# Weaving a gated-scan attention into an MLP's matmuls: k copied ahead of the angle rounding, attention's TensorE work in three groups per slot, x split ahead of the mixing, a second buffer for normalised x

## The chip, the cores and the metric

The kernel runs on one core of one Trainium2 chip. The metric is the device time of one execution in microseconds (us). PE is TensorE, ACT is ScalarE, DVE is VectorE, POOL is GpSimd and SP is the engine whose queue issues the loads and stores. Every engine works through its own instructions in the order of the program; engines wait for each other by semaphores alone.

## The reference

Three layers in a row, all in float32: an attention with a complex gate whose state is carried over time, a mixer with a token MLP and a channel MLP, and a second channel MLP behind a layer norm.

```
# attention: batch 4, heads 8, time 768, head 48
mag = sqrt(a_re**2 + a_im**2); scale = minimum(mag, 0.999) / (mag + 1e-6)
for t: S = (a_t * S) + k_t v_t^T (complex a_t, per row of S);  y_t = q_t @ S.real
x = y as [4, 768, 384]
# mixer
u = x + (relu(x^T @ w_tok1) @ w_tok2)^T          # 768 -> 256 -> 768
x2 = u + relu(u @ w_ch1) @ w_ch2                 # 384 -> 1536 -> 384
# second MLP
xn = (x2 - mean) / sqrt(var + 1e-6) * g_ln
out = x2 + relu(xn @ w2_ch1) @ w2_ch2
```

## The kernel before

**Tiles.** Time is cut into tiles of 128 steps, six (`NT`) to a batch of four, so there are 24 tiles n. For a tile, ACT and DVE compute the gate's running product (a logarithm, a scan, exponentials) and its running angle (an arctangent, a scan, a rounding, two sines), and with them "hats", q and k turned and scaled. SP lays the hats out anew (`rows<-hats`, six transfers a tile). PE then does for each half (`part`) of the eight heads: `turn_k` (k transposed into PSUM bank 6, which ACT copies to `khat`: `keep_khat`) and `scores` (q times k into PSUM bank 5, which DVE masks: `mask`); then `outputs` for each half, and `chunk_state` (DVE's `add_state` reads it). There is one bank for each, so `turn_k(n, 1)` waits for `keep_khat(n, 0)` and `scores(n, 1)` for `mask(n, 0)`. `keep_x` copies the result into the tile of x.

**Passes.** Matmuls of the MLPs have both operands split into a rounded part and a rest, and go in three passes (lines 330, 331, 332 of `split_passes`). ACT rounds (`round_x`, `relu_hidden`, `round_piece` for weights), DVE makes the rest (`rest_x`, `rest_hidden`, `rest_piece`).

**Order.** It is written out by hand for each engine. First the attention of batch 0. Then for each batch b: `mix_tokens(b)` (the token MLP and the transposes of u), and the 24 steps m of the channel MLP, `up(m)` and `down(m)`. The first three MLPs carry the attention of the next batch: one tile n = 6(b+1)+j is a **slot** j of four steps. In it PE interleaves four ups and four downs with the tile's parts; ACT and DVE call `slot`, where `step(i)` is `relu_hidden` or `rest_hidden` of step i, and `prepare(n + 1, ...)` and `prepare(n + 2, ...)` are parts of the gate for the next two tiles. Slots are n = 6 to 23: n = 6 to 11 in batch 0, 12 to 17 in batch 1, 18 to 23 in batch 2. ACT needs one set of tables for logarithm and exponential (`use_logs`) and one for arctangent and sine (`use_turns`), and loads each once a slot.

At a slot's end ACT has `log_magnitude`, `growth` and `angle` for tile n + 2, and DVE `log_sums` between them. The next slot begins on ACT with `relu_hidden(m)`, and on DVE with `rest_hidden(m)`, `turn_scan` (which waits for the arctangent) and only then `mask(n, 0)`. In the fourth slot of a batch (j = 3) DVE also does `add_u` and `row_stats`.

**Mixing.** `mix_down` needs the split of each tile of x; for batches 1 to 3 the split is made at the start of `mix_tokens`, into the space that u's split held.

**Second MLP.** For each batch, `normalise(kk, g)` writes three tiles of normalised x into `xn`, which PE transposes (`turn_xn`). The second half g = 1 uses the same `xn`, so it waits until PE has transposed the first.

Of the kernel before, what the change touches and what calls it, by code (L numbers as in the profile page):

```python
# [13 lines left out]
P = 128  # L14


def gated_scan_mixer_mlp_kernel(nc, q, k, v, a_re, a_im, w_tok1, w_tok2, w_ch1, w_ch2, g_ln, w2_ch1, w2_ch2,
# [43 lines left out]
    with ctx:  # L61
# [52 lines left out]
        raw_ch2b = alloc(m_ctx, "raw_ch2b", [P, FT * C])  # L114
        m_ctx.close()
# [65 lines left out]
        xn = by_tile(plain_tok[:, :, :].rearrange("p n c -> p (n c)")[:, 2 * COLS:2 * COLS + ST * C])  # L181
# [147 lines left out]
        def split_passes(ps, lhs_h, lhs_l, rhs_h, rhs_l, first, final):  # L329
            nc.tensor.matmul(ps, lhs_h, rhs_h, start=first, stop=False, skip_group_check=True)  # L330
            nc.tensor.matmul(ps, lhs_h, rhs_l, start=False, stop=False, skip_group_check=True)  # L331
            return nc.tensor.matmul(ps, lhs_l, rhs_h, start=False, stop=final, skip_group_check=True)  # L332

# [253 lines left out]
        def _(act):  # L587
# [107 lines left out]
            def slot(n, step, slow):  # L695
                step(0)
                prepare(n + 1, round_turns)
                keep_khat(n, 0)
                step(1)
                prepare(n + 1, sines)  # L700
                keep_khat(n, 1)
                prepare(n + 1, decays)
                step(2)
                use_logs()
                prepare(n + 2, square, inverse_of_re)
                step(3)
                prepare(n + 2, log_magnitude)
                keep_x(n, slow)
                prepare(n + 2, growth)
                use_turns()  # L710
                prepare(n + 2, angle)

            def mix_tokens(b):
                if b:
                    for j in range(NT):
                        round_x(b * NT + j)
                for rt in range(RT):
                    act.wait_ge(tok1_done, b * RT + rt + 1)
                    nc.scalar.activation(r1_h[:, rt, :], r1_ps(b)[rt][:, 0:C], ACT.Relu).then_inc(tok_hidden_rounded, 1)
                if b == 0:  # L720
                    use_logs()
                    square(5)
                    round_piece(act, 2)
                    inverse_of_re(5)
                    log_magnitude(5)
                    round_piece(act, 5)
# [4 lines left out]
                if b == 0:  # L731
                    growth(5)
                    use_turns()
                    angle(5)
# [126 lines left out]
        def _(dve):  # L861
# [95 lines left out]
            def rest_x(n):  # L957
                b, j = divmod(n, NT)
                dve.wait_ge(x_rounded, n + 1)
                nc.vector.tensor_tensor(xs_l[:, j, :], x_tile(b, j), xs_h[:, j, :].bitcast(F32), ALU.subtract).then_inc(x_split, 1)  # L960
# [6 lines left out]
            def slot(n, step):  # L967
                step(0)
# [56 lines left out]
            def normalise(kk, g):  # L1025
                b = ORDER[kk]
                dve.wait_ge(rstd_ready, 1 if kk != 1 else 2)
                if kk == 1:
                    dve.wait_ge(x2_kept, B * NT)
                else:  # L1030
                    dve.wait_ge(x2_loaded[kk % 2], 16 * NT * (1 + kk // 2) if kk % 2 == 0 else 16 * NT)
                if kk or g:
                    dve.wait_ge(xn_turned, kk * 2 * CT + g * CT)
                for st in range(ST):
                    j = g * ST + st
                    nc.vector.tensor_scalar(xn[:, st, :], x_tile(kk, j), mean_var[:, b, 2 * j:2 * j + 1], rstd_all[:, b, j:j + 1],
                                            ALU.subtract, ALU.mult).then_inc(xn_ready, 1)
# [9 lines left out]
            def mix_tokens(b):  # L1047
                if b:
                    for j in range(NT):
                        rest_x(b * NT + j)  # L1050
                    add_u(2 * b - 1)
# [17 lines left out]
                if b:  # L1069
                    row_stats(2 * b - 1)  # L1070
                else:
                    rest_piece(dve, 5)
                    log_sums(5)
# [91 lines left out]
            for m in range((B - 1) * STEPS, LAST):  # L1165
# [10 lines left out]
                if kk < 0:  # L1176
# [4 lines left out]
                    if s == 8:  # L1181
                        rstd(0, slice(0, B - 1))
                        normalise(0, 0)
                    if 12 <= s < 18:
                        rest_turned(0, s - 12)
                        if s == 14:
                            normalise(0, 1)
                    if s == STEPS - 1:
                        rest_piece(dve, 2 + PER_MLP + CT)
                else:  # L1190
# [6 lines left out]
                    if kk + 1 < B:  # L1197
                        if s == 5:
                            normalise(kk + 1, 0)
                        if 7 <= s < 13:  # L1200
                            rest_turned(kk + 1, s - 7)
                            if s == 9:
                                normalise(kk + 1, 1)
# [3 lines left out]
        def _(pe):  # L1207
# [98 lines left out]
            def turn_xn(kk, i):  # L1306
# [6 lines left out]
                for st in range(ST):  # L1313
                    last = nc.tensor.transpose(turn2_ps[ct][:, st * P:(st + 1) * P], xn[:, st, ct * P:(ct + 1) * P], ident[:, :])  # L1314
                last.then_inc(xn_turned, 1)

            def mix_down(b, rt, j):
                pe.wait_ge(x_split, b * NT + j + 1)
                last = split_passes(r1_ps(b)[rt][:, 0:C], tok1_h[:, j, rt * P:(rt + 1) * P], tok1_l[:, j, rt * P:(rt + 1) * P],
                                    xs_h[:, j, :], xs_l[:, j, :], j == 0, j == NT - 1)  # L1320
                if j == NT - 1:
                    last.then_inc(tok1_done, 1)

            def mix_tokens(b):
# [3 lines left out]
                for rt in range(RT):  # L1328
                    for j in range(NT) if b else (NT - 1,):
# [40 lines left out]
            for b in range(B):  # L1370
                mix_tokens(b)
                first = b * STEPS
                if b + 1 < B:
                    for j in range(NT):
# [17 lines left out]
                        down(m + 1)  # L1392
                        chunk_state(n)
# [67 lines left out]
```

## Time and profile before

| | |
|---|---|
| median of 3 runs | 970.07 us (969.06 to 970.95) |
| profiled execution | 970.12 us, span 968.3 us |
| PE busy | 886.5 us (92%) |
| DVE busy | 469.7 us (49%) |
| ACT busy | 414.9 us (43%) |
| POOL busy | 21.6 us (2%) |
| mean granted TensorE clock | 0.981 |

PE is busy nearly all the time, so what the time depends on is where PE stands still, and on whom it then waits. The attention of batch 0 takes the first 128 us. Weaved slots run from 142 to 555 us with two mixings between them, and after 571 us PE has only MLP steps, with the transposes of normalised x.

### The profile page before, as it was taken

To read this page: it belongs to the slowest core of one execution; us is meant where nothing else is said; L and a number is where in the kernel's file an instruction comes from. 1 tells how busy PE (TensorE), PEld (TensorE's weight loads), DVE (VectorE), ACT (ScalarE), POOL (GpSimd) and SP (SyncE) were. 2 spreads that over 40 slices of the span, in tenths; PEclk is the share of its full clock that TensorE was granted. 3 is DMA by queue.
4 is the path that set the end of the run, shared out by engine and by line. 5 is a ranking of instruction groups with operands and counts; after the bars stand their busy time and mean duration, and the time that the engine had idled before them with its cause. 6 is when DMAs were issued, how large, how long until landed. Compare 5 with 4: busy or idle time off the path is not lost.

```text
span 968.3 us, 13819 instructions
## 1 busy us (share of the span) xinstructions
PE 886.5 (92%) x5600; PEld 868.4 (90%) x5600; DVE 469.7 (49%) x821; ACT 414.9 (43%) x767; POOL 21.6 (2%) x39
## 2 busy tenths in 40 slices
PE   0768887899999999999999999899999999999998
PEld 0657777889999999989999999899999999999998
DVE  5866456656558557566665354425312322322121
ACT  6766356665655656646665332222211211211111
POOL 1000000000000000000000000000000000000000
PEclk9979897999999999999999999999999999999999
DMA  9826953434442544534436070000002002000000
GB/s 370 175 42 99 257 103 44 87 74 97 94 99 37 111 76 98 92 81 75 74 58 113 3 269 1 1 1 1 26 1 74 1 25 74 1 25 25 1 25 25
DMA packets 46834, 70.99 MB, mean 73 GB/s; under 512 B 5040, under 2 KB 38064, under 8 KB 46256
## 3 DMA queue, kind: packets, MB, share of 16 engines
q1 hardware_dynamic: 46768, 70.09, 31.2%
q8 instruction: 44, 0.72, 0.3%
q14 instruction: 22, 0.18, 0.1%
HBM read 42.86 MB, written 8.26 MB: 53 GB/s over the span
## 4 chain that ended last, share of the span: by engine, by line
PE 74%; DVE 11%; ACT 7%; DMA 4%; issue 2%; SPq 2%; DVEq 0%; ACTq 0%
PE bank L330 20%; PE bank L332 20%; PE bank L331 20%; PE bank L1229 3%; PE bank L1248 3%; DMA rows<-hats 3%; PE bank L1246 3%; PE bank L1220 2%; DMA x_u<-in_re_rows_dram 1%; PE bank L1259 1%; SPq L463 1%; ACT L594 1%; PE bank L1212 1%; DVE turned_x L1068 1%; PE bank L1314 1%
## 5 line engine op out<-in xcount | busy, mean ns | idle before, releaser
L984 DVE SCALAR_TENSOR_TENSOR hidden<-bank,hidden 128x384 fp32r<-128x384 f32 x192 | 106.9, 557 | 347.9 <-ACT hidden L693 347.8
L693 ACT ACTIVATE hidden<-bank 128x384 fp32r<-128x384 f32 x192 | 93.8, 488 | 347.8 <-PE bank L332 347.3
L330 PE MATMUL bank<-ch,hidden 128*128 128x384 f32 x576 | 198.5, 345 | 0.0
L332 PE MATMUL bank<-ch,hidden 128*128 128x384 f32 x576 | 194.1, 337 | 0.0
L331 PE MATMUL bank<-ch,hidden 128*128 128x384 f32 x576 | 193.9, 337 | 0.0
L330 PEld LDWEIGHTS bank<-ch,hidden 128*128 128x128 f32 x576 | 109.2, 190 | 0.4 <-issue 0.3
L331 PEld LDWEIGHTS bank<-ch,hidden 128*128 128x128 f32 x576 | 109.2, 190 | 0.0
L332 PEld LDWEIGHTS bank<-ch,hidden 128*128 128x128 f32 x576 | 109.0, 189 | 0.0
L330 PE MATMUL bank<-turned_x,ch 128*128 128x384 f32 x288 | 102.3, 355 | 1.9 <-DVE turned_x L1068 1.9
L332 PE MATMUL bank<-turned_x,ch 128*128 128x384 f32 x288 | 97.3, 338 | 0.0
L331 PE MATMUL bank<-turned_x,ch 128*128 128x384 f32 x288 | 97.2, 337 | 0.0
L1212 PE MATMUL bank<-ident_r 128*128 128x512 f32 x110 | 42.8, 473 | 28.8 <-DVE hats L930 28.8
L1246 PE MATMUL bank<-v_t,scratch 128*128 128x48 f32 x384 | 67.1, 266 | 0.0
L1246 PEld LDWEIGHTS bank<-v_t,scratch 128*128 128x128 f32 x384 | 62.3, 195 | 1.1
L1248 PE MATMUL bank<-state,rows 96*128 96x48 f32 x320 | 62.3, 277 | 0.0
L1220 PE MATMUL bank<-ident,rows 96*128 96x96 f32 x192 | 26.7, 264 | 33.7 <-ACT scratch L660 29.6
L330 PEld LDWEIGHTS bank<-turned_x,ch 128*128 128x128 f32 x288 | 54.7, 190 | 2.8 <-issue 2.3
L1220 PEld LDWEIGHTS bank<-ident,rows 96*128 96x128 f32 x192 | 20.3, 147 | 40.5 <-ACT scratch L660 32.2
L331 PEld LDWEIGHTS bank<-turned_x,ch 128*128 128x128 f32 x288 | 54.7, 190 | 0.0
L332 PEld LDWEIGHTS bank<-turned_x,ch 128*128 128x128 f32 x288 | 54.5, 189 | 0.0
L1229 PE MATMUL bank<-rows 96*128 96x128 f32 x384 | 54.4, 287 | 0.0
L938 DVE TENSOR_TENSOR scratch<-bank,causal 128x512 f32<-128x512 f32 x48 | 33.1, 689 | 43.2 <-PE bank L1229 43.2
(165 smaller groups left out, 1555.0 us busy)
## 6 DMA issues: line engine op xcount, KB each, us to landing
rows<-hats SPq DMA_DIRECT2D x126, 128.5 KB, 4.6
a_t<-in_a_rows_dram SPq DMA_DIRECT2D x20, 384.0 KB, 4.0
qk_t<-in_qk_rows_dram SPq DMA_DIRECT2D x19, 384.0 KB, 5.6
v_t<-in_v_cols_dram SPq DMA_DIRECT2D x24, 192.0 KB, 4.1
plain_ch<-in_moe_w_ch_dram SPq DMA_DIRECT2D x6, 768.0 KB, 10.8
out_dram<-x_u SPq DMA_DIRECT2D x24, 192.0 KB, 2.0
x_kept_dram<-x_u SPq DMA_DIRECT2D x18, 192.0 KB, 3.2
x_u<-x_kept_dram SPq DMA_DIRECT2D x18, 192.0 KB, 3.2
```

The costliest lines, as they stand in the source:

```text
L330: nc.tensor.matmul(ps, lhs_h, rhs_h, start=first, stop=False, skip_group_check=True)
L331: nc.tensor.matmul(ps, lhs_h, rhs_l, start=False, stop=False, skip_group_check=True)
L332: return nc.tensor.matmul(ps, lhs_l, rhs_h, start=False, stop=final, skip_group_check=True)
L463: sp.dma_start(rows[r * D + g * DD:r * D + (g + 1) * DD, n % 2, :, :], hats_of(n)[:, r, g, :]).then_inc(rows_landed[n % 2], 16)
L693: nc.scalar.activation(hid_h[:, m % NHID, :], hid_ps[m % 2][:, 0:HALF], ACT.Relu).then_inc(hidden_rounded, 1)
L938: nc.vector.tensor_tensor(masked[:, part * 512:(part + 1) * 512].rearrange("p (h t) -> p h t", h=HB), scored[:, :].rearrange("p (h t) -> p ...
L984: nc.vector.scalar_tensor_tensor(out=hid_l[:, m % NHID, :], in0=hid_ps[m % 2][:, 0:HALF], scalar=0.0, in1=hid_h[:, m % NHID, :].bitcast(F3 ...
L1212: nc.tensor.matmul(banks[0][:, :], ident_r[:, :], ident_r[:, :].unsqueeze(1).to_broadcast([P, 4, P]), start=True, stop=True)
L1220: last = nc.tensor.transpose(turned[:, g * D2:(g + 1) * D2], rows[:, n % 2, part * HB + g, P:2 * P], ident[0:D2, 0:D2])
L1229: last = nc.tensor.matmul(scored[:, g * P:(g + 1) * P], rows[:, n % 2, part * HB + g, P:2 * P], rows[:, n % 2, part * HB + g, 0:P], start= ...
L1246: last = nc.tensor.matmul(yh, masked[:, h * P:(h + 1) * P], v_head(n, h), start=True, stop=n % NT == 0)
L1248: last = nc.tensor.matmul(yh, rows[:, n % 2, h, 0:P], state[:, n % 2, h * D:(h + 1) * D], start=False, stop=True)
```

## The change

PE gets another order in a slot. Before, `turn_k` and `scores` of each half, the two `outputs` and `chunk_state` stood apart between ups and downs; now they stand in three groups: `turn_k` and `scores` of half 0; the same of half 1; and both `outputs` with `chunk_state`. The third `up` and `down` stand ahead of that last group, and the slot's fourth `up` behind it.

ACT copies `khat` ahead of `round_turns`, and keeps x ahead of step 3. In slot n = 6 the piece of weights 5 and the growth and angle of tile 7 move out of `mix_tokens(0)` to behind the first copy of k. DVE adds the state ahead of step 3. The split of x goes from the start of the mixing into the slots j = 3 and j = 5 (even tiles first, then, behind step 3, the odd ones), and `mix_down` goes through tiles in that order, both halves (`rt`) of each in turn. `xn` becomes two buffers, one for each half, and both halves are normalised in neighbouring steps (8 and 9, then 4 and 5).

```diff
+        xn_second = alloc(m_ctx, "xn_second", [P, ST * C])
...
+        def mix_order(b):
+            return (*range(0, NT, 2), *range(1, NT, 2)) if b else range(NT)
...
@@ ACT
             def slot(n, step, slow):
+                b, j = divmod(n, NT)
                 step(0)
-                prepare(n + 1, round_turns)
                 keep_khat(n, 0)
-                step(1)
-                prepare(n + 1, sines)
-                keep_khat(n, 1)
-                prepare(n + 1, decays)
+                if j == ST:
+                    for i in range(0, ST, 2):
+                        round_x(b * NT + i)
+                if j == NT - 1:
+                    round_x(b * NT + j - 1)
+                if n == NT:
+                    round_piece(act, 5)
+                    growth(n + 1 - PAIRS)
+                    use_turns()
+                    angle(n + 1 - PAIRS)
+                    step(1)
+                    keep_khat(n, 1)
+                    prepare(n + 1, round_turns)
+                else:
+                    prepare(n + 1, round_turns)
+                    step(1)
+                    keep_khat(n, 1)
+                prepare(n + 1, sines, decays)
                 step(2)
                 use_logs()
                 prepare(n + 2, square, inverse_of_re)
+                keep_x(n, slow)
                 step(3)
-                prepare(n + 2, log_magnitude)
-                keep_x(n, slow)
-                prepare(n + 2, growth)
+                if j == NT - 1:
+                    for i in range(1, NT, 2):
+                        round_x(b * NT + i)
+                prepare(n + 2, log_magnitude, growth)
                 use_turns()
                 prepare(n + 2, angle)
...
@@ DVE
             def slot(n, step):
+                b, j = divmod(n, NT)
                 step(0)
-                prepare(n + 1, turn_scan)
-                mask(n, 0)
-                step(1)
-                prepare(n + 1, turns_wrapped)
-                mask(n, 1)
+                if n == NT:
+                    mask(n, 0)
+                    rest_piece(dve, 5)
+                    mask(n, 1)
+                    prepare(n + 1, turn_scan)
+                    step(1)
+                    prepare(n + 1, turns_wrapped)
+                else:
+                    prepare(n + 1, turn_scan)
+                    mask(n, 0)
+                    if j == ST:
+                        for i in range(0, ST, 2):
+                            rest_x(b * NT + i)
+                    if j == NT - 1:
+                        rest_x(b * NT + j - 1)
+                    step(1)
+                    prepare(n + 1, turns_wrapped)
+                    mask(n, 1)
                 prepare(n + 1, grown_qk)
                 step(2)
                 prepare(n + 1, turn_hats)
                 prepare(n + 2, abs2)
+                add_state(n)
                 step(3)
+                if j == NT - 1:
+                    for i in range(1, NT, 2):
+                        rest_x(b * NT + i)
                 prepare(n + 2, ratio0, ratio_step, log_sums)
-                add_state(n)
...
@@ PE
-                for rt in range(RT):
-                    for j in range(NT) if b else (NT - 1,):
+                for j in mix_order(b) if b else (NT - 1,):
+                    for rt in range(RT):
                         mix_down(b, rt, j)
...
                         turn_k(n, 0)
+                        scores(n, 0)
                         up(m + 1)
-                        scores(n, 0)
                         turn_k(n, 1)
+                        scores(n, 1)
                         if j:
                             down(m - 1)
-                        scores(n, 1)
                         up(m + 2)
+                        down(m)
                         outputs(n, 0)
-                        down(m)
+                        outputs(n, 1)
+                        chunk_state(n)
                         up(m + 3)
-                        outputs(n, 1)
                         down(m + 1)
-                        chunk_state(n)
```

On PE, in a slot in the middle of batch 1's MLP, these rows stood before (L1220 is `turn_k`, L1229 `scores`, L1246 `outputs`, L1259 `chunk_state`; an `up` reads `turned_x`, a `down` reads `hidden`; of each group the first row):

```order
L1220 MATMUL bank<-ident,rows 128x96 [waits khat_kept,rows_landed0]
...
L330 MATMUL bank<-turned_x,ch 128x384 [waits hidden_split]
...
L1229 MATMUL bank<-rows 128x128 [waits state_sums]
...
L1220 MATMUL bank<-ident,rows 128x96 [waits khat_kept]
...
L1229 MATMUL bank<-rows 128x128 [waits scores_masked]
...
L1246 MATMUL bank<-v_t,scratch 128x48 [waits states_decayed,scores_masked,x_kept,loaded_v0]
...
L1259 MATMUL bank<-v_t,scratch 96x48 [waits khat_kept,scores_masked]
```

And these stand there now (L1248 is `turn_k`, L1257 `scores`, L1274 `outputs`, L1287 `chunk_state`):

```order
L1248 MATMUL bank<-ident,rows 128x96 [waits khat_kept,rows_landed0]
...
L1257 MATMUL bank<-rows 128x128 [waits state_sums]
...
L331 MATMUL bank<-turned_x,ch 128x384 [waits hidden_split]
...
L1248 MATMUL bank<-ident,rows 128x96 [waits khat_kept]
...
L1257 MATMUL bank<-rows 128x128 [waits scores_masked]
...
L1274 MATMUL bank<-v_t,scratch 128x48 [waits states_decayed,scores_masked,x_kept,loaded_v0]
...
L1287 MATMUL bank<-v_t,scratch 96x48 [waits khat_kept,scores_masked]
L331 MATMUL bank<-turned_x,ch 128x384 [waits hidden_split]
```

The first scores moved ahead of an up, the second scores ahead of a down, and the slot's last up from ahead of the second outputs to behind the chunk's state.

On ACT, from the end of one slot into the next, these rows stood before (L624 is `growth`, L632 `angle`, L693 the ReLU, L637 `round_turns`, L660 `keep_khat`):

```order
L672 ACTIVATE x_u<-bank 128x384 [waits outputs_ready]
L624 ACTIVATE grow<-scratch 128x384 [waits grown,log_sums_done]
L625 ACTIVATE grow<-scratch 128x384
L594 ACT_TABLE_LOAD
L632 ACTIVATE scratch<-scratch 128x384 [waits hats_done,ratio_done]
L693 ACTIVATE hidden<-bank 128x384 [waits hidden_used,hidden_ready]
L637 ACTIVATE scratch<-scratch,round_bias 128x384 [waits turn_sums]
L660 ACTIVATE scratch<-bank 128x384 [waits k_turned]
```

And these stand there now (the same operations, at L632, L640, L701, L668 and L645; L680 is `keep_x`):

```order
L680 ACTIVATE x_u<-bank 128x384 [waits outputs_ready]
L701 ACTIVATE hidden<-bank 128x384 [waits hidden_used,hidden_ready]
...
L632 ACTIVATE grow<-scratch 128x384 [waits grown,log_sums_done]
L633 ACTIVATE grow<-scratch 128x384
L602 ACT_TABLE_LOAD
L640 ACTIVATE scratch<-scratch 128x384 [waits hats_done,ratio_done]
L701 ACTIVATE hidden<-bank 128x384 [waits hidden_used,hidden_ready]
L668 ACTIVATE scratch<-bank 128x384 [waits k_turned]
L645 ACTIVATE scratch<-scratch,round_bias 128x384 [waits turn_sums]
```

The copy of k moved ahead of the rounding, and x is kept one step earlier; growth, table load, angle and the next slot's first ReLU stand in the order in which they stood.

## Rows read from the trace of the kernel before

**Rows 1.** Waits of PE over the whole span: total, times, longest in us

```profile
PE bank L1220 <- ACT scratch L660: 29.6, 10, 8.3
...
PE bank L1314 <- DVE plain_tok L1036: 6.6, 4, 2.7
...
PE bank L1220 <- DMA rows<-hats: 4.0, 5, 1.5
PE bank L330 <- DVE turned_x L960: 3.9, 3, 1.8
...
PE bank L330 <- DVE hidden L1054: 0.6, 1, 0.6
```

**Rows 2.** Timeline of PE around slot n = 14: start, duration, tile, shapes, count

```profile
333.55 0.42 PE L330 MATMUL bank<-turned_x,ch 128*128 128x384 f32 x1
...
349.07 0.32 PE L1246 MATMUL bank<-v_t,scratch 128*128 128x48 f32 x2
...
353.73 0.42 PE L330 MATMUL bank<-turned_x,ch 128*128 128x384 f32 x1
...
356.94 0.49 PE L1220 MATMUL bank<-ident,rows 96*128 96x96 f32 x4
...
361.85 1.06 PE L1229 MATMUL bank<-rows 96*128 96x128 f32 x8
```

**Rows 3.** Timeline of ACT over the same slot's end

```profile
349.27 0.49 ACT L693 ACTIVATE hidden<-bank 128x384 fp32r<-128x384 f32 x1 [1.32 <-PE bank L332]
...
353.56 0.52 ACT L624 ACTIVATE grow<-scratch 128x384 f32<-128x384 f32 x1 [1.24 <-DVE scratch L893]
...
354.52 1.28 ACT L594 ACT_TABLE_LOAD   x1
355.81 0.52 ACT L632 ACTIVATE scratch<-scratch 128x384 f32<-128x384 f32 x1
356.24 0.47 ACT L693 ACTIVATE hidden<-bank 128x384 fp32r<-128x384 f32 x1
...
359.32 0.47 ACT L660 ACTIVATE scratch<-bank 128x384 f32<-128x384 f32 x1
```

**Rows 4.** Timeline of DVE over the same slot's end

```profile
351.97 0.56 DVE L888 SCALAR_TENSOR_TENSOR scratch<-scratch 128x384 f32<-128x384 f32 x1
...
357.81 0.96 DVE L905 TENSOR_TENSOR_SCAN scratch<-keep,scratch 128x384 f32<-128x384 f32 x1
360.05 0.69 DVE L938 TENSOR_TENSOR scratch<-bank,causal 128x512 f32<-128x512 f32 x1 [1.29 <-PE bank L1229]
```

**Rows 5.** Timeline: the tile's hats on DVE, and PE's wait for their rows

```profile
368.46 1.81 DVE L930 TENSOR_TENSOR hats<-qk_t,scratch 128x768 f32<-128x768 f32 x2
...
378.02 0.55 PE L1220 MATMUL bank<-ident,rows 96*128 96x96 f32 x4 [0.74 <-DMA rows<-hats]
```

**Rows 6.** Timeline of PE in batch 0's MLP: first up, two waits, the tenth tile's slot

```profile
142.28 0.44 PE L330 MATMUL bank<-turned_x,ch 128*128 128x384 f32 x1 [0.19 <-DVE turned_x L1068]
...
153.06 0.90 PE L1220 MATMUL bank<-ident,rows 96*128 96x96 f32 x4 [6.10 <-ACT scratch L660]
...
200.24 0.90 PE L1220 MATMUL bank<-ident,rows 96*128 96x96 f32 x4 [2.36 <-ACT scratch L660]
...
215.83 0.42 PE L330 MATMUL bank<-turned_x,ch 128*128 128x384 f32 x1
```

**Rows 7.** Timeline of ACT and DVE there: a piece of weights rounded, and its rest

```profile
153.27 1.48 ACT L322 ACTIVATE ch<-plain_ch 128x1536 fp32r<-128x1536 f32 x1
...
154.79 1.76 DVE L327 TENSOR_TENSOR ch<-plain_ch,ch 128x1536 fp32r<-128x1536 f32 x1 [0.81 <-ACT ch L322]
```

**Rows 8.** Stretches: length, busy of PE, PEld, DVE, ACT, POOL, granted clock, DMA

```profile
202.00:204.00 2.00, 2.00 (x10) 2.00 (x8) 0.00 (x0) 1.78 (x6) 0.00 (x0) 0.59 0.00 0
280.00:282.00 2.00, 1.09 (x6) 1.12 (x7) 1.79 (x4) 2.00 (x6) 0.00 (x0) 1.00 0.00 0
618.00:619.00 1.00, 0.67 (x5) 0.68 (x6) 0.27 (x1) 0.00 (x0) 0.00 (x0) 1.00 0.00 0
```

More of the change, by code:

```diff
@@ L332, in split_passes, with splits_through @@
             return nc.tensor.matmul(ps, lhs_l, rhs_h, start=False, stop=final, skip_group_check=True)
+        def mix_order(b):
+            return (*range(0, NT, 2), *range(1, NT, 2)) if b else range(NT)
+        def splits_through(n):
+            b, j = divmod(n, NT)
+            return b * NT + list(mix_order(b)).index(j) + 1
         def links(n):
@@ L713, in mix_tokens @@
             def mix_tokens(b):
-                if b:
-                    for j in range(NT):
-                        round_x(b * NT + j)
                 for rt in range(RT):
@@ L730, in mix_tokens @@
                     nc.scalar.activation(u_h[:, ct, g * HALF:(g + 1) * HALF], turn_ps[i][:, 0:HALF], ACT.Copy).then_inc(u_rounded, 1)
[L731 to L734, printed above, removed]
             def log_variances(i, bs):
@@ L958, in rest_x @@
                 b, j = divmod(n, NT)
-                dve.wait_ge(x_rounded, n + 1)
+                dve.wait_ge(x_rounded, splits_through(n))
                 nc.vector.tensor_tensor(xs_l[:, j, :], x_tile(b, j), xs_h[:, j, :].bitcast(F32), ALU.subtract).then_inc(x_split, 1)
@@ L967, in slot @@
             def slot(n, step):
+                b, j = divmod(n, NT)
                 step(0)
[L969 to L973 removed]
+                if n == NT:
[16 more added lines that the diff above has]
+                    mask(n, 1)
                 prepare(n + 1, grown_qk)
@@ L1031, in normalise @@
                     dve.wait_ge(x2_loaded[kk % 2], 16 * NT * (1 + kk // 2) if kk % 2 == 0 else 16 * NT)
-                if kk or g:
-                    dve.wait_ge(xn_turned, kk * 2 * CT + g * CT)
+                if kk:
+                    dve.wait_ge(xn_turned, (kk - 1) * 2 * CT + (g + 1) * CT)
                 for st in range(ST):
                     j = g * ST + st
-                    nc.vector.tensor_scalar(xn[:, st, :], x_tile(kk, j), mean_var[:, b, 2 * j:2 * j + 1], rstd_all[:, b, j:j + 1],
+                    nc.vector.tensor_scalar(xn[g][:, st, :], x_tile(kk, j), mean_var[:, b, 2 * j:2 * j + 1], rstd_all[:, b, j:j + 1],
                                             ALU.subtract, ALU.mult).then_inc(xn_ready, 1)
@@ L1048, in mix_tokens @@
                 if b:
-                    for j in range(NT):
-                        rest_x(b * NT + j)
                     add_u(2 * b - 1)
@@ L1183, in _ @@
                         normalise(0, 0)
+                    if s == 9:
+                        normalise(0, 1)
                     if 12 <= s < 18:
                         rest_turned(0, s - 12)
-                        if s == 14:
-                            normalise(0, 1)
                     if s == STEPS - 1:
@@ L1197, in _ @@
                     if kk + 1 < B:
-                        if s == 5:
-                            normalise(kk + 1, 0)
+                        if s in (4, 5):
+                            normalise(kk + 1, s - 4)
                         if 7 <= s < 13:
                             rest_turned(kk + 1, s - 7)
-                            if s == 9:
-                                normalise(kk + 1, 1)
             add_x2(4 * B - 1)
@@ L1313, in turn_xn @@
                 for st in range(ST):
-                    last = nc.tensor.transpose(turn2_ps[ct][:, st * P:(st + 1) * P], xn[:, st, ct * P:(ct + 1) * P], ident[:, :])
+                    last = nc.tensor.transpose(turn2_ps[ct][:, st * P:(st + 1) * P], xn[g][:, st, ct * P:(ct + 1) * P], ident[:, :])
                 last.then_inc(xn_turned, 1)
             def mix_down(b, rt, j):
-                pe.wait_ge(x_split, b * NT + j + 1)
+                pe.wait_ge(x_split, splits_through(b * NT + j))
                 last = split_passes(r1_ps(b)[rt][:, 0:C], tok1_h[:, j, rt * P:(rt + 1) * P], tok1_l[:, j, rt * P:(rt + 1) * P],
```

4 lines of the change are left out of this document (1 added, 3 removed).

## The prediction

> **What bounds the kernel now.** I read the view of waits first. PE, busy 92% of the span, is what the time hangs on, so only what PE waits for and what it has to issue counts. The waits that this change touches [rows 1]: 29.6 us on `keep_khat` (line 660), 6.6 us on normalised x (line 1036), 4.0 us on the transfers of the hats, 3.9 us on the split of x (line 960). Part of the 29.6 us stands in the attention of batch 0, where nothing changes: in the slots it is 6.10 and 2.36 us in n = 6 and 8 [rows 6], a wait between these in n = 7, and under 1 us each in the first two slots of batches 1 and 2.
>
> Next I read the timelines of PE, ACT and DVE over one regular slot. Slot n = 14 begins 20.18 us after n = 13 (333.55 to 353.73) [rows 2], with no wait of PE. I count from E, the end of a slot's fourth `up`; before, that is 349.07. From E on runs a chain over two engines: the ReLU at E+0.20 [rows 3]; the logarithms on ACT, and on DVE at E+2.90 the sums [rows 4]; growth at E+4.49, the table load at E+5.45, the arctangent at E+6.74, the next slot's ReLU at E+7.17 [rows 3]; on DVE the rest of hidden and the scan of angles at E+8.74 [rows 4]. The scan lasts 0.96 and its successor can start 0.87 after it, so `mask(n, 0)` could start at **E+9.61**. Its row has it at 360.05 (E+10.98), after waiting 1.29 us for PE: before the change, this chain has 1.3 us to spare there, and `scores(n, 1)`, which needs the mask done, starts at E+12.78 (361.85) [rows 2].
>
> **The change, part by part.**
>
> *PE's new order (the term that decides).* E, the end of the fourth up, now lies only one `down` (1.56 us: nine matmuls at 0.1735; 18 of them and a slow first take 3.21 in rows 2, 353.73 to 356.94) ahead of the next slot, where before 4.66 us of outputs, down and chunk lay between (349.07 to 353.73) [rows 2]. The chain from E keeps its length, since nothing in it is moved: ACT has growth, load, arctangent and ReLU in the same order, and DVE still has `turn_scan` ahead of `mask(n, 0)`. What PE does from E: down, up, down, to E+4.69 (1.56 and that 3.21, less the 0.09 of the slow first); `turn_k` and `scores` of half 0 in 1.2; up 1.65. So `turn_k(n, 1)` is wanted at E+7.54. It needs `keep_khat(n, 0)`, which ACT can only begin behind the ReLU of E+7.17: 0.37 later, and 0.47 long [rows 3], done at E+8.0. **PE waits 0.5 us.** The transposes take 0.34; `scores(n, 1)` is wanted at E+8.4. It needs the mask: E+9.61 and 0.69 [rows 4] with a little for the semaphore, E+10.35. **PE waits 1.95 us.** Then scores 0.82, down 1.65, up 1.56, down 1.56, both outputs and chunk 4.83, up 1.65: the next E is E+22.45. Nothing between can absorb it, for the next chain starts at that E. The slot's own work shrinks a little, see below, but its pitch goes from 20.18 to 22.45: **+2.28 us a slot**, 2.45 of waits less 0.2.
>
> This holds where the slot ahead prepares a tile and its fourth step is close: n = 9, 10, 11; 13 to 17; 19 to 22. That is 12 slots: **+27.4 us**. Slots 12 and 18 stand behind a mixing, where the chain has long ended, and no tile 24 is prepared ahead of slot 23. `keep_khat` ahead of `round_turns` does take away the rounding from k's path, as it should, but what is late next is the mask of scores.
>
> *Waits that go or are covered.* In these slots and in 12 and 18, before had waits of 0.73, 0.74 and 1.47 on the hats' rows, 0.96 twice and 0.61 and 0.56 on `keep_khat` (their sums stand, with others, in [rows 1]). The hats in j = 3 come later now, behind `add_u`; from their start to PE's transpose it takes 9.56 us [rows 5]. I place them at E+19.15, so their rows come 1.55 us late in slot j = 4, but this wait lies inside the 2.45 us that PE would stand there anyway. Gone: 5.3 us, less 0.35 us that slots 12 and 18 each may keep, already taken off. **-5.3 us.**
>
> *Fewer groups.* Behind attention's matmuls the first of an up or down takes 0.26 to the next start where others take 0.174. There were six such returns in a slot, there are three: -0.26; joined groups start 0.06 slower. 0.2 net is in the pitch above; slots 12, 18 and 23 get it too: **-0.8 us**.
>
> *Slots 6 to 8.* Before, the up of slot 6 starts at 142.28 and slot 9 at 215.83 [rows 6]. I walk the queues with the same durations, and 1.4 us on ACT and 1.7 us on DVE for each piece of weights [rows 7]. In slot 6 the copy of k no longer stands behind growth, load, arctangent and rounding, so the 6.10 us go, and slot 7 could begin at 157.5 and not 166.6. But the hats of tile 7 (start 156.0, rows 9.5 later) then make PE wait from 160.7 to 165.5, and the chain with its pieces lets the second scores of slot 7 start at 171.6 (before 179.5) and of slot 8 at 196.65 (before 203.8). Slot 9 starts at 210.3: **-5.5 us**. Pieces stand ahead of `log_magnitude` here, which is why less is won than the first wait promises.
>
> *The mixing.* PE's 1.77 us wait for the split of x in batches 1 and 2 goes (3.9 with one of batch 0) [rows 1]. In batch 3 there was none. But going through both `rt` for each tile ends both sums together, where before the second's 3.1 us of matmuls covered the ReLU and rest of the first; with no such cover batch 0 shows 0.63 us [rows 1], now paid three times, with 0.1 for a slower first matmul. 2 x 1.77 less 3 x 0.7: **-1.5 us**. The moved ops themselves (six of about 0.5 us on ACT and on DVE each batch) lie ahead of `add_u`'s wait and behind the fourth step, where both engines have room; the odd tiles' three delay the chain into a mixing, which waits for nothing of it.
>
> *Second buffer.* PE's four waits on line 1036 go: **-6.6 us** [rows 1]. `normalise` moves up a step and may wait for x2's loads there, but DVE has over 2 us idle in each of these steps. Unused room costs nothing.
>
> *The clock.* A wait can be followed by half speed. After the 2.36 us at 200.24 the granted clock was 0.59 [rows 6, 8]: transposes and an up took 3.53 us where 2.0 is usual, 1.5 us lost. After 2.7 us, PE's longest on line 1036 [rows 1], it was 1.00 at 618, and after the 1.77 us for the split of x too, at 281 [rows 8]. The new waits, 0.5 and 1.95 with 0.34 of work between, stand between these. I take one drop in slot 8 and one in four of the 12 slots (an estimate from those rows; bounds none and all, 0 and 18): **+6.0 us**.
>
> *Sum.* 27.4 - 5.3 - 0.8 - 5.5 - 1.5 - 6.6 + 6.0 = +13.7 on a span of 968.3, so 982.0; with 1.8 us around the span (970.12 profiled, as good as the median 970.07) 983.8, and I say **983**, as the walk of batches 1 and 2 by itself comes out about 1 us lower.
>
> **Two rules beside this.** The row shows a table load of 1.28 us and the arctangent 1.29 us after its start [rows 3]. The Trainium skill, "ScalarE: Activation LUTs", section "What ACT_TABLE_LOAD costs", adds a drain of about 1.38 us to each switch; by it the chain would be longer by 1.4 us and the sum by 12 x 1.4. The trace does not bear it out here, and the sum goes by the row. The Trainium skill, "Perfetto Trace Analysis", section "Matmul Optimizations", wants matmuls back to back in batches, which speaks for three groups; it is rival B.
>
> **Rivals.**
> A, the forecast: PE waits for the mask in 12 slots. 0.72.
> B: the grouping works and the chain does not bind. For it: the named wait is always on `keep_khat`, whose rounding is gone. Against it: E+9.61 in rows 4. It decides if the mask can be done by E+8.4, that is if the chain is 2 us shorter. Then 12 x 2.45 and the clock's 6.0 drop out: about 948. 0.12.
> C: the clock drops after nearly every wait, 9 more at 1.5: about 996. Whether it does is not told by rows at either side. 0.10.
> D: half of the chain's lateness is taken up (the mask E+9.4 or so): about 968 to 971. 0.06.
>
> The range holds A (972 to 991: one drop in four to two in three, pitch 22.45 give or take 0.3), most of D's edge and half of C: 970 to 994. Differences under 0.2% can't be told from no change; slower 0.83, same 0.04, faster 0.13.
>
> **What would show it.** Right: in regular slots PE's wait moves from `keep_khat` to the mask (the second scores waiting about 2 us for DVE), a pitch of about 22.4 us, slot 9 starting near 210, the waits on line 1036 gone, the second MLP 4 to 7 us shorter, a half-clock stretch in some slots. Wrong: if `mask(n, 0)` starts earlier than 9 us after the fourth up, or slots keep 20 us, the sum turns to B.

## The result and the profile after

The change makes the kernel slower: 1017.48 us (median of 4, 1007.97 to 1020.70) against 970.51 us, a ratio of 1.047 with a 95% interval of 1.040 to 1.054. Forecast were 983 us and a range of 970 to 994. The profiled execution, the slowest of the four, has a span of 1018.9 us, 50.6 more than before, and a granted clock of 0.934 where before had 0.981. In what follows each ratio leaves out executions more than 1.5% above the fastest of their kernel (two of seven in e2, one of four in e4), and the medians do not.

The page of the changed kernel, its span, busy time and granted clock in 40 slices:

```profile
span 1018.9 us, 13819 instructions
...
PE 931.2 (91%) x5600; PEld 909.4 (89%) x5600; DVE 468.8 (46%) x821; ACT 415.6 (41%) x767; POOL 21.6 (2%) x39
...
PEclk9978898888899897999788889999999999999999
```

PE is busy 44.7 us longer for as many instructions, DVE and ACT are not. Same matmuls, more time: that is the clock. A span times what is missing from its mean clock is 1018.9 x 0.066 = 67 us after and 968.3 x 0.019 = 18 us before: 49 of the 50.6 us. Every mark of 7 or 8 behind slice 5 lies in the slots.

The waits of PE in the changed kernel, total, times, longest (line 1248 is `turn_k`, 1257 `scores`, 954 `mask`; they answer to [rows 1]):

```profile
PE bank L1257 <- DVE scratch L954: 20.9, 15, 1.7
PE bank L1248 <- ACT scratch L668: 19.3, 9, 8.3
PE bank L1248 <- DMA rows<-hats: 6.7, 3, 5.5
PE bank L331 <- DVE hidden L1085: 2.9, 4, 0.7
```

The waits on normalised x and on the split of x are gone, and a new one is there, 15 times, for the mask. PE's timeline in slot n = 16, from the transposes of half 0, with the slot's two waits (they answer to [rows 2]):

```profile
404.66 0.49 PE L1248 MATMUL bank<-ident,rows 96*128 96x96 f32 x4
404.99 1.08 PE L1257 MATMUL bank<-rows 96*128 96x128 f32 x8
405.83 0.42 PE L331 MATMUL bank<-turned_x,ch 128*128 128x384 f32 x1
...
408.05 0.55 PE L1248 MATMUL bank<-ident,rows 96*128 96x96 f32 x4 [0.40 <-ACT scratch L668]
410.30 2.08 PE L1257 MATMUL bank<-rows 96*128 96x128 f32 x8 [1.71 <-DVE scratch L954]
```

ACT and DVE at the same place (they answer to [rows 3, 4]):

```profile
405.41 1.28 ACT L602 ACT_TABLE_LOAD   x1
406.71 0.52 ACT L640 ACTIVATE scratch<-scratch 128x384 f32<-128x384 f32 x1
407.14 0.47 ACT L701 ACTIVATE hidden<-bank 128x384 fp32r<-128x384 f32 x1
407.51 0.48 ACT L668 ACTIVATE scratch<-bank 128x384 f32<-128x384 f32 x1
```

```profile
407.64 0.56 DVE L1017 SCALAR_TENSOR_TENSOR hidden<-bank,hidden 128x384 fp32r<-128x384 f32 x1 [3.22 <-ACT hidden L701]
...
408.70 0.96 DVE L921 TENSOR_TENSOR_SCAN scratch<-keep,scratch 128x384 f32<-128x384 f32 x1
409.58 0.67 DVE L954 TENSOR_TENSOR scratch<-bank,causal 128x512 f32<-128x512 f32 x1
```

On ACT the load, the arctangent, the ReLU and the copy of k follow each other without a gap. On DVE the rest of hidden (407.64) has waited 3.22 us for that ReLU, and behind it come two short steps, the scan and the mask. PE's scores, wanted at 408.6, start as the mask ends. The other regular slots repeat it.

What the waits don't tell is in the granted clock. Four stretches of the same kernel: the end of a slot's last group, what follows it, and the wait above (columns as in [rows 8]):

```profile
341.00:345.00 4.00, 4.00 (x37) 4.00 (x35) 2.47 (x4) 2.76 (x4) 0.00 (x0) 1.00 0.32 73
345.00:346.00 1.00, 1.00 (x10) 1.00 (x10) 0.00 (x0) 0.49 (x1) 0.00 (x0) 0.69 1.15 130
346.00:350.00 4.00, 4.00 (x18) 4.00 (x18) 0.55 (x1) 0.00 (x0) 0.84 (x1) 0.50 1.15 124
...
410.00:412.00 2.00, 1.70 (x8) 1.70 (x9) 1.44 (x4) 1.29 (x4) 0.00 (x0) 0.56 0.00 0
```

And PE's timeline around the first of them, the joined group of slot n = 13:

```profile
341.55 0.32 PE L1274 MATMUL bank<-v_t,scratch 128*128 128x48 f32 x2
...
345.05 2.46 PE L1287 MATMUL bank<-v_t,scratch 128*96 128x48 f32 x16
347.30 0.67 PE L331 MATMUL bank<-turned_x,ch 128*128 128x384 f32 x1
```

At 345.4 the clock falls to its lower level, 1.2 GHz, while PE is busy without a gap: it has been at the outputs and the chunk, matmuls of 48 columns, since 341.55. The last wait, the slot's 1.71 us for the mask, ended at 335.87, 9.5 us ahead. At 410 it is the other case, a fall at the waits on k and the mask.

I summed, over stretches of half a microsecond from 130 us on to the last matmul, length times what is missing from the granted clock. Before loses 8.5 us in three stretches, all in or behind the three long waits of slots 6 to 8 (6.10, 3.27 and 2.36 us). The changed kernel loses 54.6 us in 22: 25.6 us in 11 stretches that begin in or behind a wait, and **29.0 us in 11 that begin in a joined group or right behind it**. In the changed kernel most of these groups have a wait on the mask some 10 us ahead, so this count alone does not clear the waits. The experiments do.

### The profile page after: what moved, and what is told of

The parts are those of the page before. It is cut to its first block, busy times and chain, and to the rows that moved or that the text cites. A ratio compares the mean times of both kernels' runs of the same rounds, so it can differ in the third digit from the quotient of the medians.

```text
span 1018.9 us, 13819 instructions
## 1 busy us (share of the span) xinstructions
PE 931.2 (91%) x5600; PEld 909.4 (89%) x5600; DVE 468.8 (46%) x821; ACT 415.6 (41%) x767; POOL 21.6 (2%) x39
## 4 chain that ended last, share of the span: by engine, by line
PE 75%; DVE 10%; ACT 9%; issue 4%; DMA 2%; SPq 0%; DVEq 0%; ACTq 0%
PE bank L331 20%; PE bank L333 20%; PE bank L332 20%; PE bank L1257 3%; PE bank L1274 3%; PE bank L1276 3%; PE bank L1287 3%; ACT L602 2%; PE bank L1240 2%; DMA x_u<-in_re_rows_dram 1%; DVE scratch L954 1%; ACT hidden L701 1%; DVE scratch L909 1%; DVE turned_x L1099 1%; ACT grow L633 1%
## 5 line engine op out<-in xcount | busy, mean ns | idle before, releaser
L701 ACT ACTIVATE hidden<-bank 128x384 fp32r<-128x384 f32 x192 | 93.7, 488 | 394.2 <-PE bank L333 393.9
L331 PE MATMUL bank<-ch,hidden 128*128 128x384 f32 x576 | 201.8, 350 | 0.1
L332 PE MATMUL bank<-ch,hidden 128*128 128x384 f32 x576 | 199.0, 345 | 0.0
L333 PE MATMUL bank<-ch,hidden 128*128 128x384 f32 x576 | 198.6, 345 | 0.0
L331 PEld LDWEIGHTS bank<-ch,hidden 128*128 128x128 f32 x576 | 114.5, 199 | 0.7 <-issue 0.7
L332 PEld LDWEIGHTS bank<-ch,hidden 128*128 128x128 f32 x576 | 113.8, 198 | 0.0
L333 PEld LDWEIGHTS bank<-ch,hidden 128*128 128x128 f32 x576 | 113.1, 196 | 0.0
L331 PE MATMUL bank<-turned_x,ch 128*128 128x384 f32 x288 | 109.2, 379 | 1.9 <-DVE turned_x L1099 1.9
L332 PE MATMUL bank<-turned_x,ch 128*128 128x384 f32 x288 | 104.1, 361 | 0.0
L333 PE MATMUL bank<-turned_x,ch 128*128 128x384 f32 x288 | 103.7, 360 | 0.0
L1257 PE MATMUL bank<-rows 96*128 96x128 f32 x384 | 62.4, 313 | 21.2 <-DVE scratch L954 20.9
L1257 PEld LDWEIGHTS bank<-rows 96*128 96x128 f32 x384 | 55.5, 220 | 25.9 <-DVE scratch L954 25.4
L1274 PE MATMUL bank<-v_t,scratch 128*128 128x48 f32 x384 | 67.6, 268 | 0.0
L331 PEld LDWEIGHTS bank<-turned_x,ch 128*128 128x128 f32 x288 | 60.6, 210 | 2.8 <-issue 2.3
L1274 PEld LDWEIGHTS bank<-v_t,scratch 128*128 128x128 f32 x384 | 60.4, 193 | 1.1
L332 PEld LDWEIGHTS bank<-turned_x,ch 128*128 128x128 f32 x288 | 60.2, 209 | 0.0
L333 PEld LDWEIGHTS bank<-turned_x,ch 128*128 128x128 f32 x288 | 59.9, 208 | 0.0
L1240 PEld LDWEIGHTS bank<-ident_r 128*128 128x128 f32 x110 | 23.4, 218 | 31.6 <-issue 28.9
L1248 PEld LDWEIGHTS bank<-ident,rows 96*128 96x128 f32 x192 | 20.8, 147 | 33.8 <-ACT scratch L668 23.7
```

The source lines that it names most:

```text
L701: nc.scalar.activation(hid_h[:, m % NHID, :], hid_ps[m % 2][:, 0:HALF], ACT.Relu).then_inc(hidden_rounded, 1)
L1240: nc.tensor.matmul(banks[0][:, :], ident_r[:, :], ident_r[:, :].unsqueeze(1).to_broadcast([P, 4, P]), start=True, stop=True)
L1248: last = nc.tensor.transpose(turned[:, g * D2:(g + 1) * D2], rows[:, n % 2, part * HB + g, P:2 * P], ident[0:D2, 0:D2])
L1257: last = nc.tensor.matmul(scored[:, g * P:(g + 1) * P], rows[:, n % 2, part * HB + g, P:2 * P], rows[:, n % 2, part * HB + g, 0:P], start= ...
L1274: last = nc.tensor.matmul(yh, masked[:, h * P:(h + 1) * P], v_head(n, h), start=True, stop=n % NT == 0)
```

## The experiments

Each kernel was timed in three rounds beside the kernel before on the same chip; "lost" is the clock's sum just described, of the profiled execution.

**e1, outputs apart.** TensorE of the changed kernel:

```diff
                         up(m + 2)
-                        down(m)
                         outputs(n, 0)
+                        down(m)
                         outputs(n, 1)
                         chunk_state(n)
```

> The changed kernel with one edit on TensorE: outputs(n, 0) stands ahead of down(m) again, so that the last group of a slot is outputs(n, 1) with chunk_state(n) alone and the 48-column matmuls no longer stand in one run of 4.8 us. The fourth up stays behind the chunk, so the late mask stays. Theory N (the clock falls because the narrow matmuls stand in one run, with no wait ahead of it): the eleven or so stretches of half clock that begin in or behind that group go (some 25 to 30 us lost there in the changed kernel's trace), the waits of 1.7 us on the mask stay, and the time is about 985 to 992. Theory W (the clock falls because of the waits alone, and the stretches behind the group are their late effect): nothing goes, about 1010 to 1020.

Measured 998.58 us, ratio 1.029 (1.024 to 1.034), span 991.3, lost 22.2 us in 11 stretches. Every one begins in or behind a wait: the 11 of the joined group are gone, with their 29.0 us, and what lies at waits is 22.2 us where it was 25.6. The waits on the mask stay:

```profile
349.01 1.16 PE L1257 MATMUL bank<-rows 96*128 96x128 f32 x8 [1.70 <-DVE scratch L954]
```

Theory N holds for what lay behind the group, and W, the waits alone, falls. The time is 7 us above what I had written down. Part of that are the waits for the hats' rows, 10.6 us where the changed kernel has 6.7.

**e2, mask first.** VectorE of the changed kernel, in all slots but n = 6:

```diff
+                mask(n, 0)
                 step(0)
                 prepare(n + 1, turn_scan)
-                mask(n, 0)
```

> The changed kernel with one edit on VectorE: in every slot but n = 6 mask(n, 0) stands ahead of rest_hidden(m) and turn_scan. The chain from the fourth up no longer holds the mask; only the wait of about 0.4 us for the copy of k is left in a regular slot. Theory W: both the waits (some 20 us) and nearly all the lost clock go, about 955 to 965. Theory N: the waits and the half clock behind them go (some 20 us and 15 to 20 us), but the stretches behind the joined group stay: about 975 to 990.

978.87 us, ratio 1.002 (0.997 to 1.007), span 974.4, lost 25.6 us. No wait on the mask is left, that for k is 0.26 to 0.41 us in six regular slots, and those for the hats' rows have grown from 6.7 to 12.2 us. The span is 44.5 us shorter than that of the changed kernel (38.6 by the medians). This is N's number. The place of one instruction of 0.69 us is worth that much because of what waits for it and what the clock does then. Nine of its 11 stretches at half clock begin in or right behind the joined group.

**e3, joined group in the kernel before.** TensorE of before:

```diff
                         up(m + 2)
-                        outputs(n, 0)
                         down(m)
                         up(m + 3)
+                        outputs(n, 0)
                         outputs(n, 1)
-                        down(m + 1)
                         chunk_state(n)
+                        down(m + 1)
```

> The kernel before with one edit on TensorE: the fourth up is moved ahead of both outputs, and outputs(n, 0), outputs(n, 1) and chunk_state(n) stand in one group, down(m + 1) behind it. The fourth up lies earlier than in the changed kernel, so the mask is in time and no wait is added. Theory N: the clock falls in or behind the joined group in most of the 18 slots, 1.7 to 3.4 us lost each time: 985 to 1010. Theory W: no wait, no fall: 967 to 971.

979.71 us, ratio 1.009 (1.005 to 1.014), span 977.9, lost 29.0 us where before lost 8.5. Of the 29.0 us, 18.8 lie in eight stretches in or right behind the joined group, the rest at long waits (5.1, 1.7 and, at the 2.7 us for normalised x, 3.4). So the group costs time with no late mask anywhere. The time is under N's range: the clock fell in eight slots of 18 and not in most, and the earlier ups shortened other waits by 7.2 us. Those on k are 1.94 and 1.02 us in slots 7 and 8, and of the two of 1.77 us for the split of x only 0.36 us is left.

**e4, all but the groups.** The changed kernel with TensorE's slots in the order of before.

> The changed kernel with the order of TensorE's slots of the kernel before (the three groups undone), all else as changed: copy of k ahead of the rounding, piece 5 and the growth of tile 7 moved, x split in the slots, pairs of row blocks for each tile in the mixing, second buffer for normalised x. Both theories say that the loss lies in the groups alone: 6.6 us less in the second MLP, some 1 to 2 us less in the mixing, 4 to 10 us less in slots 6 to 8: 950 to 960.

A miss: 997.73 us, ratio 1.024 (1.021 to 1.027), lost 25.6 us. PE waits about 2.36 us for k in nearly every slot. ACT, DVE and PE of this kernel show why:

```profile
338.83 0.49 ACT L680 ACTIVATE x_u<-bank 128x384 f32<-128x384 f32 x1 [3.04 <-PE bank L1276]
339.22 0.49 ACT L701 ACTIVATE hidden<-bank 128x384 fp32r<-128x384 f32 x1
...
346.56 0.52 ACT L632 ACTIVATE grow<-scratch 128x384 f32<-128x384 f32 x1 [4.69 <-DVE scratch L909]
...
349.61 0.48 ACT L668 ACTIVATE scratch<-bank 128x384 f32<-128x384 f32 x1
```

```profile
341.79 0.55 DVE L967 TENSOR_TENSOR state_sum<-bank,state 96x384 f32<-96x384 f32 x1 [6.33 <-PE bank L1287]
342.26 0.54 DVE L1017 SCALAR_TENSOR_TENSOR hidden<-bank,hidden 128x384 fp32r<-128x384 f32 x1
```

```profile
350.15 0.55 PE L1248 MATMUL bank<-ident,rows 96*128 96x96 f32 x4 [2.36 <-ACT scratch L668]
```

Two moves of the change stand wrong for PE's old order. On ACT, `keep_x` stands ahead of the fourth ReLU and waits for the second outputs, which come behind the fourth up here: 3.04 us. On DVE, `add_state` (L967) stands ahead of the rest of the fourth hidden and waits 6.33 us for the chunk, which comes last in PE's old slot. DVE is the later of the two: ACT's growth stands idle for another 4.69 us until DVE's sums are there, and comes 9.64 us behind the end of the fourth up (336.92) where before took 4.49. Both moves belong to PE's new order, and the expectation overlooked them.

**e5, the keeps back too.** e4 with

```diff
+                step(3)
+                prepare(n + 2, log_magnitude)
                 keep_x(n, slow)
-                step(3)
...
-                prepare(n + 2, log_magnitude, growth)
+                prepare(n + 2, growth)
```

and `add_state` at the slot's end on VectorE.

> As the run with TensorE's order of before, and with two more moves undone that belong to it: keep_x stands behind log_magnitude again and add_state at the slot's end, where before had them (the odd tiles' split behind them). Kept of the change: copy of k ahead of the rounding, the moves in slot 6, x split in the slots and the mixing's order, second buffer. Theory K (the 2.36 us waits of that run come from keep_x ahead of the fourth ReLU, which waits for the second outputs and so makes the chain of growth, angle and mask start late): these waits go in all slots, little half clock is left, about 953 to 960. Rival (copying k ahead of the rounding is itself what makes k late): the waits stay, 990 or more.

947.54 us, ratio 0.975 (0.970 to 0.980): faster than before, and over 5 us below my range for theory K. In slots 7 to 23 only the first of a batch waits for the mask (0.52 us) and the hats' rows cost 4.9 us in slot 7 and 0.35 to 1.2 in four others. Lost: 3.4 us, in one stretch. The rival falls: copying k first is not what makes it late. That `keep_x` is, as theory K has it, is not shown: the run put both moves back at once, and by e4's rows it was `add_state` that ended last. Neither was put back alone. The profiled execution is the slowest of the five, 955.02 us. Its first up starts at 150.47, 8 us later than before's, and it lost 18.8 us of clock in its first 130 us where before lost 10.2. So a difference of some 8 us between executions can lie in the attention of batch 0, where nothing was changed.

**e8, row blocks apart.** e5 with the mixing's loops turned back:

```diff
-                for j in mix_order(b) if b else (NT - 1,):
-                    for rt in range(RT):
+                for rt in range(RT):
+                    for j in mix_order(b) if b else (NT - 1,):
                         mix_down(b, rt, j)
```

> The kernel of the run before this one, with the mixing's first sums made one row block after the other again (even tiles first in each), so that the ReLU and rest of the first lie under the second's matmuls. The three waits of 0.74 us at the second weights' first matmul go in batches 1 to 3: 2.2 to 2.7 us less than that run. Rival: the time only moves to the next wait of the mixing (the transposes), no difference.

943.79 us, ratio 0.972 (0.967 to 0.977), span 941.9, lost 1.7 us; its four times lie within 0.5 us. The page's first lines and PE's wait at the second weights:

```profile
span 941.9 us, 13819 instructions
...
PE 879.3 (93%) x5600; PEld 863.9 (92%) x5600; DVE 469.0 (50%) x821; ACT 417.1 (44%) x767; POOL 21.6 (2%) x39
...
PE bank L331 <- DVE hidden L1086: 0.7, 1, 0.7
```

e5 has three more such waits, 2.2 us in all, and they are gone, as expected. The medians differ by 3.75 us. From the first up to the end the profiled executions differ by 3.1, and the clock lost 1.7 us less in e8's, which can be the rest. This is the fastest version, ahead of both kernels.

**e6, second buffer alone**, in the kernel before.

> The kernel before with the second buffer for normalised x alone, both halves normalised in neighbouring steps. PE's four waits on it go, 6.6 to 7 us less: 963 to 964, ratio 0.993. Rival (the transposes only meet the next wait, on the split of turned x or on the loads of x): 966 to 970.

963.37 us, ratio 0.992 (0.988 to 0.996), span 961.6 with 8.5 us lost as before: 6.7 us less, as expected.

**e7, both repairs.** The changed kernel with the edits of e1 and e2.

> The changed kernel with both edits that were tried apart: mask(n, 0) ahead of rest_hidden and turn_scan on VectorE, and outputs(n, 0) ahead of down(m) on TensorE. Theory N and W together: with no wait on the mask and no run of narrow matmuls longer than 3 us, the clock stays at full speed in nearly all slots (under 10 us lost in all, where the changed kernel lost 55), waits of under 0.5 us on k and 1 to 2 us on the hats' rows stay in some: 952 to 962. If the outputs split still loses over 15 us of clock, the length of the narrow run is not what counts.

962.90 us, ratio 0.992 (0.989 to 0.995), lost 6.8 us in four stretches, each behind a wait for the hats' rows. Groups of scores with k are kept here, and so is the second outputs' with the chunk, a run of 3.06 us; no stretch begins in them. It stays 19 us of span behind e8: its waits on k, the hats' rows and the mask come to 35.3 us where e8 has 24.7, those in the mixing to 2.9 where e8 has 0.7, and it lost 5.1 us more of clock. So even without the long run the groups cost time.

**e9 and e10, how long a run.** e8 with the order of e3, and with `down(m + 1)` between the second outputs and the chunk.

> The fastest kernel so far (TensorE's order of before, row blocks apart, 943.8 us, 1.7 us of clock lost) with one edit on TensorE: the fourth up goes ahead of both outputs, and outputs(n, 0), outputs(n, 1) and chunk_state(n) stand in one run of 4.8 us. No wait is added, as the up comes earlier. Theory N (a long run of narrow matmuls by itself brings the clock down): half-clock stretches beginning in or right behind the run in a part of the 18 slots, 10 to 30 us lost, 952 to 972, and a spread between runs of over 3 us. Rival (it takes a wait near the run as well): under 4 us lost, 941 to 946.

> As the run before, but with a down between the outputs and the chunk: the longest run of narrow matmuls is 3.4 us, not 4.8. Theory N, by the length of the run: fewer stretches, 0 to 10 us lost, 942 to 953. If it loses as much as the run of 4.8 us, the length beyond 3.4 us does not matter; if nothing, the chunk's joining is what brings the clock down.

e9: 969.93 us (964.33 to 973.11), ratio 0.998 (0.996 to 1.000), lost 27.3 us in ten stretches. One of them, with no wait of PE over 0.15 us for the 50 us ahead of it:

```profile
223.00:228.00 5.00, 5.00 (x42) 5.00 (x41) 4.53 (x9) 4.24 (x8) 0.00 (x0) 1.00 0.07 17
228.00:229.00 1.00, 1.00 (x13) 1.00 (x13) 1.00 (x3) 0.94 (x3) 0.00 (x0) 0.95 0.79 188
229.00:232.00 3.00, 3.00 (x14) 3.00 (x14) 2.53 (x5) 1.73 (x5) 0.00 (x0) 0.50 1.15 122
```

Its waits are no longer than e8's, for the hats even shorter (6.5 us in all, e8 8.3):

```profile
PE bank L1249 <- ACT scratch L668: 14.8, 3, 8.3
PE bank L1249 <- DMA rows<-hats: 6.5, 2, 5.4
```

e10: 947.37 us (944.70 to 953.07), ratio 0.977 (0.972 to 0.981), lost 8.5 us in four stretches, three of them behind no wait. So the rival falls (a wait is not needed), and the run's length counts. In e9 the run is 4.85 us long in 12 of the 18 slots, and the clock fell in or right behind nine of these. It is shorter in a batch's first slot (3.06 us, no state yet to multiply) and in its last (3.49 us, no chunk), and there the clock did not fall. In e10 the run is 3.49 us long in 15 slots, and the clock fell in three. At e8's runs of 1.70 us it fell in none.

**e11, k first alone**, in the kernel before (`keep_khat` ahead of `round_turns` and of the sines).

> The kernel before with one edit on ScalarE: keep_khat(n, 0) ahead of round_turns and keep_khat(n, 1) ahead of the sines, slot 6's other moves left out. The waits of 3.27 and 2.36 us in slots 7 and 8 and of 0.96 and 0.6 in batches 1 and 2 go or shrink to under 0.5, that of 6.10 us in slot 6 shrinks to 3 to 4 (k still behind growth, load and angle), and the clock lost behind them goes in part: 8 to 14 us less, 957 to 963. Rival: the hats' rows come no sooner, so half of it comes back as waits on the transfers, 964 to 968.

960.38 us, ratio 0.989 (0.987 to 0.991), within 0.6 us from run to run, lost 5.1 us: 10 us less, 3.4 of them the clock's. The waits on k in slots 7, 8, 12, 13, 18 and 19 are gone, and those for the hats' rows have grown from 4.0 to 6.4 us. Slot 6 waits 3.40 for k and 1.35 for the mask where it waited 6.10.

## Why the prediction was wrong

**The step that failed** is the term of the clock: "I take one drop in slot 8 and one in four of the 12 slots", +6.0 us, with the sentence ahead of it, "A wait can be followed by half speed". It let only waits lower the clock. The changed kernel loses 46 us more than before where 6.0 was put down. 29.0 of its 54.6 us stand behind the joined outputs and chunk, which the prediction had only as a gain of 0.2 us a slot; e1, e3 and e9 show that this run of 48-column matmuls does it without any wait. The other 25.6 us stand behind waits, in 9 of the 12 regular slots where I had taken a quarter, and in slots 7 and 8, and each cost 1.7 or 3.4 us, not 1.5. Before's own trace has three falls, at its waits of 6.10, 3.27 and 2.36 us, and the prediction names only the last. Rival C had the direction, at 996, but the same blind spot.

**The waits: right in kind, a little large.** Forecast were 0.5 us for k and 1.95 for the mask in slots 9 to 11, 13 to 17 and 19 to 22. The wait on the mask is there in all 12, 1.70 or 1.71 us in eight and 1.06 to 1.53 in the others. That on k is 0.29 to 0.40 us in five, and does not show in the rest. E+9.61 and the order of the chain hold to a tenth. The pitch from slot 14's scores at 360.68 to slot 15's at 383.19, both behind the mask, with no clock lost between, is 22.51 us; forecast 22.45. Rivals B and D fall.

**The sum without its clock.** It was +7.7. The changed span less its 54.6 us is 964.3, before's less its 8.5 is 959.8: +4.5, of which 1.5 lies ahead of the first up, where this execution lost 11.9 us of clock in its first 130 us and before's 10.2. The waits of the 12 slots come to 21.0 us where 12 x 2.45 = 29.4 was forecast. Clock that is lost while PE stands in a wait costs nothing, so losses and waits do not add up to the microsecond.

**Slots 6 to 8.** The first wait went from 6.10 to none for k, and one for the hats' rows came, forecast 4.8, measured 5.51, with 3.4 us of clock lost at it that the forecast had not put down. I had slot 9 start 5.5 us earlier; in the trace it starts at 216.75 (before 215.83), with the first up of batch 0 at 143.79, 1.5 later than before. That is 0.6 us less between the two, with 10.3 us of clock lost there.

**The mixing and the buffer.** The waits for the split of x went; 0.74 us came at the second weights three times (forecast 0.63). The stretch from the first up behind the last mixing to the end shows the buffer, in the changed kernel:

```profile
628.72:1018.90 390.18, 385.79 (x2232) 384.25 (x2232) 122.48 (x248) 80.91 (x156) 0.00 (x0) 1.00 0.07 22
```

and before:

```profile
570.59:968.30 397.71, 386.76 (x2232) 384.06 (x2232) 122.28 (x248) 80.84 (x156) 0.00 (x0) 1.00 0.07 23
```

That is 7.5 us less, and e6 has the same 390.3 there; 6.6 was forecast.

**What the change was worth.** Its parts other than the three groups and what belongs to them, e5, are worth -23 us; the copy of k ahead of the rounding alone -10 (e11), the second buffer -7 (e6). The groups, with the moves of `keep_x` and `add_state` that belong to them, add 70 and so make +47 of it.

## What to carry to other kernels

When narrow matmuls are gathered into one group, ask what the clock does with the longer run, not only what the switches cost: here two runs of 1.7 us and one of 1.3 cost nothing, and one of 4.85 us cost 2.7 us of clock on average in nine slots of 12. When a step is moved later on the engine that sets the pace, walk the whole chain that starts from it, over all queues, to the first thing that the pace-setter needs from it. And moves on one engine (`keep_x` and `add_state` ahead of the slot's fourth step) can be right for one order of another engine only, so undo them together, and look on every engine for the wait that ends last: in e4 it was DVE's, though PE waited for ACT.

## What the runs showed of the hardware

The granted clock fell to half with TensorE busy all the time. The changed kernel, e2, e3 and e9 have one run of 48-column matmuls in each slot. In or right behind a run of 4.85 us it fell in 9, 7, 6 and 9 slots of 12, behind one of 3.49 us (a batch's last slot) in 2, 2, 2 and 0 of 3, and behind one of 3.06 us (a batch's first) in none. In e10 it fell in 3 of 15 runs of 3.49 us, in e1 and e7 in none of the 12 of 3.06 us that each has, and in e8 in none of 1.70 us. Whether it is their 48 columns or the weights that each of these matmuls loads was not tried apart.

The stretches at half clock lost 1.7 us each or 3.4, and 5.1 at the wait of 6.1 us in slot 6 (before, e3, e6), nothing between. A wait of one length can go either way: that of 2.7 us on normalised x lost nothing in before, 3.4 us in e3 and 1.7 in e11.

How much is lost changes from execution to execution, and so does the time: e9's ten have granted clocks from 0.948 to 0.959 and times spread over 8.8 us, e8's four spread over 0.5. The Trainium skill, "Perfetto Trace Analysis", section "Matmul Optimizations", asks for matmuls back to back in batches because the engine scales with utilization. In e8 and in e9 alike the slots' matmuls stand back to back, and for these narrow ones the traces show the opposite of gathering: apart, between wide matmuls, they kept the full clock.
